# Attention with two feed-forward blocks: the denominator's inversion behind the spread of the maxima in the first batch, and each batch's first projections at its front

## The reference

```python
def phi(x):                                   # x @ w_phi, 128 features
    proj = np.einsum('bhsd,df->bhsf', x, w_phi)
    proj = proj - np.max(np.abs(proj), axis=-1, keepdims=True)
    return np.concatenate([np.exp(proj), np.exp(-proj)], axis=-1)
q_p, k_p = (phi(q), phi(k))
kv = np.einsum('bhsf,bhsd->bhfd', k_p, v)
z = np.sum(k_p, axis=2)
num = np.einsum('bhsf,bhfd->bhsd', q_p, kv)
den = np.einsum('bhsf,bhf->bhs', q_p, z)[..., None] + 1e-06
x = num / den                                 # heads side by side: (B, S, 512)

xk = mu_k * x + (1.0 - mu_k) * x_prev         # x_prev: x one token earlier
xr = mu_r * x + (1.0 - mu_r) * x_prev
k = np.maximum(xk @ w_k, 0.0)
y = 1.0 / (1.0 + np.exp(-(xr @ w_r))) * (k * k @ w_v)

h = np.maximum(y @ w_in, 0.0)
conv_out = ...                                # three taps along the tokens
out = h * sigmoid(conv_out) @ w_out
```

## Time and profile before

| | us |
|---|---|
| median of 3 executions | 1399.35 |
| lowest, highest | 1394.55, 1399.78 |
| the profiled execution | 1397.19 |
| its span, first to last instruction | 1395.3 |
| TensorE busy | 1333.8 (96%) |
| VectorE busy | 756.6 (54%) |
| ScalarE busy | 599.2 (43%) |

### The profile page before, as it was taken

How to read it: one execution, slowest core, us unless ns; L and a number is a source line. 1 busy time by engine, 2 the same in 40 slices (tenths; PEclk the granted TensorE clock), 3 DMA queues, 4 the chain that set the end, 5 groups by cost and what they waited for, 6 DMA issues and landing times. The chain is left out here.

```text
span 1395.3 us, 25154 instructions
## 1 busy us (share of the span) xinstructions
PE 1333.8 (96%) x9720; PEld 1192.8 (85%) x9720; DVE 756.6 (54%) x1275; ACT 599.2 (43%) x1079; POOL 13.1 (1%) x18
## 2 busy tenths in 40 slices
PE   8779999999999999999999999998899999999998
PEld 7559898889888888888888888998798998998997
DVE  6557355545654544644565455451855755754853
ACT  3345445354353533534435344352533443533532
POOL 0000000000000000000000000000300000000000
PEclk9879999999999999999999999999999999999999
DMA  4421202202212111220221221221110110110101
GB/s 136 141 62 41 59 27 79 64 18 80 62 36 71 50 50 42 66 71 15 76 62 37 71 54 50 73 70 48 65 65 31 43 65 31 41 64 32 40 30 38
DMA packets 92657, 78.56 MB, mean 56 GB/s; under 512 B 62736, under 2 KB 71056, under 8 KB 91536
## 3 DMA queue, kind: packets, MB, share of 16 engines
q1 hardware_dynamic: 92560, 77.09, 18.4%
HBM read 57.75 MB, written 19.02 MB: 55 GB/s over the span
## 5 line engine op out<-in xcount | busy, mean ns | idle before, releaser
L459 PE MATMUL psm<-xk_hi,wk_hi 128*128 128x288 f32 x512 | 154.4, 302 | 14.5 <-issue 7.1
L982 PE MATMUL psh<-y_hi,win_hi 128*128 128x288 f32 x512 | 154.8, 302 | 13.4 <-ACT h L1067 9.0
L830 DVE TENSOR_TENSOR k_lo<-square,k_hi 128x288 fp32r<-128x288 f32 x128 | 58.5, 457 | 195.1 <-ACT square L677 194.8
L983 PE MATMUL psh<-y_lo,win_hi 128*128 128x288 f32 x512 | 153.1, 299 | 0.0
L459 PE MATMUL psm<-k_hi,wv_hi 128*128 128x288 f32 x512 | 152.8, 299 | 0.0
L984 PE MATMUL psh<-y_hi,win_lo 128*128 128x288 f32 x512 | 152.5, 298 | 0.0
L459 PE MATMUL psm<-xk_lo,wk_hi 128*128 128x288 f32 x512 | 152.2, 297 | 0.0
L459 PE MATMUL psm<-k_lo,wv_hi 128*128 128x288 f32 x512 | 152.0, 297 | 0.0
L459 PE MATMUL psm<-xk_hi,wk_lo 128*128 128x288 f32 x512 | 151.9, 297 | 0.0
L459 PE MATMUL psm<-k_hi,wv_lo 128*128 128x288 f32 x512 | 151.7, 296 | 0.0
L1125 DVE SCALAR_TENSOR_TENSOR conv<-h,taps,conv 128x576 f32<-128x576 f32 x64 | 55.2, 862 | 143.2 <-ACT conv L1069 143.2
(11 more groups left out here) (130 smaller groups left out, 2900.4 us busy)
## 6 DMA issues: line engine op xcount, KB each, us to landing
v_nat<-in_v SPq DMA_DIRECT2D x32, 320.0 KB, 3.6
qk<-in_q SPq DMA_DIRECT2D x32, 288.0 KB, 3.3
qk<-in_k SPq DMA_DIRECT2D x32, 288.0 KB, 3.7
den<-den_scr SPq DMA_DIRECT2D x64, 144.0 KB, 3.0
y_scr<-y SPq DMA_DIRECT2D x64, 144.0 KB, 2.0
y<-y_scr SPq DMA_DIRECT2D x8, 1152.0 KB, 5.6
out<-rows SPq DMA_DIRECT2D x32, 256.0 KB, 2.0
stage<-in_moe_w_in SPq DMA_DIRECT2D x4, 512.0 KB, 3.2
```

What stands on the lines that cost most here:

```text
L459: return nc.tensor.matmul(o, lhsT, rhs, start=first, stop=last, skip_group_check=True)
L830: nc.vector.tensor_tensor(k2_lo[:, i, :], square[:, i % 2, :], k2_hi[:, i, :].bitcast(F32), ALU.subtract).then_inc(k2_lo_ready, 1)
L982: nc.tensor.matmul(o, wh, xh, start=first, stop=False, skip_group_check=True)
L983: nc.tensor.matmul(o, wh, xl, start=False, stop=False, skip_group_check=True)
```

## The change

In the first batch's list RC of the pair before moves from ahead of M to behind KV, and DV from behind PICK to the next pair's E, QT and EK (two pairs later than its own), ahead of NUM. In every other block `FIRST_FILL` becomes 0, so E(0) is the block's first step and all tiles come later in relation to attention. DV of pair 0 is held back until the last mix of x of the other half has been put out.

```diff
-FIRST_FILL, RC_AFTER, DV_AFTER = 4000, 2500, 8500
+FIRST_FILL, RC_AFTER, DV_AFTER = 0, 2500, 8500
...
-        def before(*names):
-            return [(s, p - 1) for s in names] if p else []
-
-        steps += [("E", p), ("QT", p), ("EK", p)] + before("DEN", "NUM") + [("WARM", p)] + before("RC")
-        steps += [("M", p), ("KV", p), ("PICK", p)] + before("DV")
+        def of(q, *names):
+            return [(s, q) for s in names] if q >= 0 else []
+
+        steps += [("E", p), ("QT", p), ("EK", p)] + of(p - 2, "DV") + of(p - 1, "DEN", "NUM") + [("WARM", p)]
+        steps += [("M", p), ("KV", p)] + of(p - 1, "RC") + [("PICK", p)]
     p = PAIRS - 1
-    steps += [("DEN", p), ("NUM", p), ("XK", 2, 0), ("HK", 2, 0), ("LK", 2, 0), ("RC", p)]
+    steps += [("DV", p - 1), ("DEN", p), ("NUM", p), ("XK", 2, 0), ("HK", 2, 0), ("LK", 2, 0), ("RC", p)]
...
-        while later and later[0][0] <= now:
-            out.append(later.pop(0)[1])
+        due = [t for t in later if t[0] <= now and (t[1] != ("DV", 0) or ("XR", 1, 1) in out)]
+        for t in due:
+            later.remove(t)
+            out.append(t[1])
```

## The result

The changed kernel takes 1480.34 us in the median of four runs (1473.93 to 1483.81), the kernel before, run beside it, 1396.95 (1392.69 to 1399.78). The ratio is 1.0594 with a 95% interval of 1.0545 to 1.0643. I had forecast 1458 with a range of 1424 to 1474 and a chance of 0.93 for slower: the sign was right and the waits came at the places named, but the size was not right, and the time lies above the range.

The account below looks back on a forecast made before the run. TensorE, busy 1333.8 us of a 1395.3 us span, was taken as the bound; -7.3 + 27.8 + 11.4 + 7.0 + 18.2 + 4 = +61.1 on the profiled execution's 1397.2 us gave 1458 us, range 1424 to 1474.

Parts of the forecast that it names:

- a: Batch fronts: E(0) waits 5.2 to 6.6 us for k's load, 37.3 us at six fronts; cost +27.8 us.
- b: Behind the six front waits the granted clock falls to half, losing 1.9 us each: +11.4 us, bounds 0 and 20.
- c: Pair 0, seven batches: TensorE stalls 1.0 us at K tile 3 for ScalarE: +7.0 us, bounds 0 and 12.
- d: Pair 1, seven batches: mixes on VectorE make M(1) 2.4 us late, PICK(1) 0.2 more: +18.2 us, bounds 4 to 22.
- e: Pair 1, seven batches: half clock behind the wait at M(1): +4 us, bounds 0 and 8.5.
- f: First batch: PICK waits 0.35, 2.0 and 2.0 us, E(0) may start at 89.3; 7.3 us gained, bounds 3 and 11.
- clock worse: Rival: whole half-speed stretches at the fronts, one at M(1) each time, M(1) delay term at 22: 1475 us, chance 0.13.
- Only the fronts cost: Rival: VectorE and ScalarE keep up, so c, d and e are nought: 1429 us (1418 to 1440), chance 0.25.

Follow-up runs that it names:

- The early load: Changed kernel with q and k loads of the next batch's pair 0 issued ahead of the y stores, last loop pass written out: 1433.25 us, 1.0286 of before.
- the run with early load and mixes ahead: Changed kernel with pair 0's q and k loads issued ahead of the y stores and XK(1,0) ahead of DEN(0) on VectorE: 1388.90 us, 0.9969 of before.
- the run with filled waits: Changed kernel with eight 128x128 identity matmuls ahead of M(1) in every block with attention: 1443.45 us, 1.0356 of before.
- The two delay kernels: Kernel before with one or two unused 1.22 us VectorE reductions ahead of pair 1's queries: 1402.93 us (1.0062) and 1432.06 us (1.0259).
- the mixes alone in the kernel before: Kernel before with mixes XK(1,0) between pair 1's keys and queries on VectorE, that mix's remaining steps behind the queries: 1465.86 us, 1.0498 of before.
- the one with two more reductions: Kernel before with two unused reductions (2.44 us) on VectorE ahead of pair 1's queries in every block with attention: 1432.06 us, 1.0259 of before.
- the one with the fronts alone: Kernel before with only FIRST_FILL = 0, projections at each block's front, first batch's list as before: 1483.52 us, 1.0624 of before.
- first batch alone: Kernel before with only the first batch's new list, FIRST_FILL at 4000: 1385.04 us, 0.992 of before.
- first batch with early load: First batch's new list with pair 0's q and k loads issued ahead of the y stores, 4000 ns of tiles ahead of E(0): 1384.06 us, 0.9921 of before.

## Why the prediction was wrong

- **a, the queue at the front: right.** Forecast 37.3 us of waits at six fronts, measured 36.4; against the idle time there before, +26.9 for +27.8. The early load shows the cause.
- **b, the clock at the fronts: right in kind, a little small in size.** Five fronts have 6.83 us at 0.50, one 3.41. The prediction let the clock fall 2.3 to 3.4 us after a wait began; at the fronts it fell 4.6 to 4.9 us after, so at five of them 5.2 to 5.4 us of the stretch lay on work, where the forecast had 2.7 to 5.0. E(0) took 4.96 us there for 2.84. From E(0) to K tile 3, its wait left out, these fronts took 10.0 to 10.15 us and the first 9.2, for 7.8 in the run with early load and mixes ahead, which has full clock there: some 13 us for 11.4.
- **c, ScalarE at K tile 3: right in kind, about half in size.** Waits of 0.43 to 1.05 us, 4.0 in all for 7.0; where E(0) runs at half clock the K tiles come later, and less is left of the wait.
- **d, VectorE at pair 1: right in the wait, too dear in the sum.** 14.4 us of waits at M(1) for 16.8; the 0.2 at PICK(1) did not come, and the waits of 0.26 to 1.04 us that PICK(1) had before are gone, 3.6 us in all, which the forecast did not credit. So +11 for +18.2.
- **e, the clock at pair 1: this is the step that failed.** The prediction had 3.41 us at half clock behind such a wait and took half of that, +4 with a bound of 8.5. There were 13.65 us of it in six batches of seven. From M(1) to E(2), PICK's wait left out, the work took 6.2 to 6.4 us longer in these six and 4.8 in the seventh, 43 us in all. Less the 3 us that the two short stretches cost the kernel before, that is +40 for the forecast's +4; the run with filled waits gives 37 in the whole time. The rows I had sized it by were waits of 0.70 and 1.04 us **behind** KV, at PICK(1), with the V tiles following PICK at once. The new wait was two to three times as long and stood **ahead of** KV. I read a price from one place and used it at another, and I set the upper bound from the same two rows. The trace of before had a row against that bound: the wait of 0.87 us at PICK(3) of the first batch, at 79.87 in the earlier trace rows, has 6.83 us at half clock behind it, twice what I took for the worst (TensorE idles another 2.46 us within it).

```profile
80.66:87.49 6.83, 4.37 (x23) 1.12 (x24) 3.19 (x5) 2.28 (x4) 0.00 (x0) 0.50 0.12 44
```

The two delay kernels show how the length counts: 0.69 us was followed by half clock once in seven times, 1.83 us all seven times in the profiled execution.
- **f, the first batch: right.** Forecast waits 0.35, 2.0 and 2.0 us at PICK, measured 0.45, 2.19 and 1.90; the load of k to let E(0) start at 89.3, measured 90.57. M(0) of the next batch comes 8.1 us earlier, where the forecast had 7.3.

The terms as measured add up to some 86 us of the 86.7 by which the span grew.

With e at its measured size the forecast's own sum gives 1458 + 36 = 1494; c and d were 10 us too dear, which by luck hid a part of it. The rival "clock worse" (1475) was nearest, but its extra was put at the fronts. "Only the fronts cost" was refuted by the mixes alone in the kernel before.

The Trainium skill ("DMA: Bandwidth & Descriptors", Anatomy of one DMA) gives its figures for transfers that GpSimd issues, while SyncE issues these, so the 2.7 us for 288 KB is an estimate from a neighbouring case. By it the front's wait would be 4.7 us; this case's trace does not agree, with 6.0 to 6.5 us at the five fronts behind a jump, and bears out the landings measured in place, 3.2 to 4.5 us.

Open is why the stretch is long there. At M(1) KV and PICK stand between the wait and the next tiles, and in the traces the clock came back within those tiles; that what stands there decides the length is argued and not shown, since no run had a wait of 2 us at M(1) with tiles right behind it. The nearest are the waits at the loop's jump with K tiles behind them: of the seven that lasted 1.80 to 2.14 us in the profiled executions, three were followed by 3.41 us at half clock and four by none. Nor is the stretch at M(1) always so long. The changed kernel, the one with two more reductions, the one with the fronts alone and the one with the early load have 28 waits of 1.83 to 2.08 us at M(1) in all: 24 have 10.24 or 13.65 us at half clock behind them, three have 6.83, and one, of 2.08 us, none. What decides between these is not shown either.

## What to carry to other kernels

Before work is moved to the front of a loop's body, look in every queue for what it needs. Where its load is issued by the new pass, behind the old pass's last store, the tiles that stood in front hid that load. A short wait of the bounding engine must be priced together with what its clock does afterwards, and that price belongs to the place: take it from a wait of the same length in front of the same work, and where there is none, bound it by all the work that follows up to where a trace shows the clock back. And a step has a place on every engine: the mixes made the queries 2.5 us late on VectorE, and when they were moved behind the queries, KV waited 4 us by way of ScalarE.

## What the runs showed of the hardware

- At M(1), in front of KV, waits of TensorE of 1.83 to 2.08 us were followed by 10.24 or 13.65 us at 1.2 GHz 24 times of 28 (profiled executions of the changed kernel, of the fronts alone, of the early load and of the two more reductions). Waits of 0.69 us at the same place were followed by half clock once in seven times, for 6.83 us.
- Waits of 1.25 to 2.14 us at the loop's jump with K tiles behind them were followed by none 26 times of 29 and by 3.41 us three times (kernel before, first batch alone, mixes between, both delays, first batch with early load); the three are waits of 1.80, 1.91 and 2.00 us.
- Eight matmuls of an identity (1.95 us) in place of the idle time at M(1) kept the clock at 2.4 GHz there in all seven batches. Of the 54 us that the place of XK(1,0) was worth in seven batches, 37 were the clock and 14.4 the waits.
- A load of k of 288 KB that SyncE issued behind the last store of y landed 3.2 to 4.5 us later in the kernel before.
